# One small VectorE instruction in place of two, in the softmax of an attention stage

## The reference

```python
q_bits = (np.einsum('bhsd,dk->bhsk', q, proj) > 0)      # B, H, S, D = 2, 8, 768, 64; 6 bits
k_bits = (np.einsum('bhsd,dk->bhsk', k, proj) > 0)
mask = q_bucket[:, :, :, None] == k_bucket[:, :, None, :]
scores = np.where(mask, scale * np.matmul(q, k.transpose(0, 1, 3, 2)), -1000000000.0)
scores = scores - np.max(scores, axis=-1, keepdims=True)
attn = np.exp(scores)
attn = attn / (np.sum(attn, axis=-1, keepdims=True) + 1e-09)
return np.matmul(attn, v)
```

## Time and profile before

| | us |
|---|---|
| median of three runs | 738.78 |
| the profiled execution | 738.64 |
| its span, first to last instruction | 736.8 |
| PE busy | 712.6 (97%) |
| DVE busy | 410.8 (56%) |
| ACT busy | 340.2 (46%) |
| POOL busy | 322.7 (44%) |

### The profile page before, as it was taken

How to read it: one execution, slowest core, us unless ns; L and a number is a source line. 1 busy time by engine, 2 the same in 40 slices (tenths; PEclk the granted TensorE clock), 3 DMA queues, 4 the chain that set the end, 5 groups by cost and what they waited for, 6 DMA issues and landing times.

```text
span 736.8 us, 10909 instructions
## 1 busy us (share of the span) xinstructions
PE 712.6 (97%) x3754; PEld 604.0 (82%) x3754; DVE 410.8 (56%) x827; ACT 340.2 (46%) x689; POOL 322.7 (44%) x283
## 2 busy tenths in 40 slices
PE   3999999999999999999999999999999999999998
PEld 2788898889888877888888888888888888888876
DVE  2998899889989587833131122211343556845443
ACT  1899999999999644333101111111233334223101
POOL 3798888878888257955100000020034555121100
PEclk9999999999999999999999999999999999999999
DMA  6464753333332012522000001020011220000002
GB/s 167 115 158 116 179 133 95 104 104 97 95 80 55 1 44 87 152 69 80 1 0 1 1 0 43 2 78 1 1 43 44 86 56 24 1 28 16 15 28 86
DMA packets 39400, 45.77 MB, mean 62 GB/s; under 512 B 15796, under 2 KB 26676, under 8 KB 39348
## 3 DMA queue, kind: packets, MB, share of 16 engines
q1 hardware_dynamic: 36564, 41.65, 20.6%
q0 software_dynamic: 2784, 3.43, 1.8%
HBM read 28.16 MB, written 3.15 MB: 42 GB/s over the span
## 4 chain that ended last, share of the span: by engine, by line
PE 79%; DVE 12%; issue 4%; ACT 2%; DMA 1%; POOL 1%; SPq 1%; ACTq 0%; POOLq 0%; DVEq 0%
PE PS L890 21%; PE PS L892 21%; PE PS L891 21%; DVE negmax L1235 5%; DVE ETL L1244 3%; PE PS L981 3%; PE PS L1021 3%; PE PS L1006 2%; PE PS L1007 2%; PE PS L1022 2%; PE PS L1109 1%; DVE bias L1237 1%; ACT E L775 1%; ACT OS L787 1%; PE PS L992 1%
## 5 line engine op out<-in xcount | busy, mean ns | idle before, releaser
L1387 DVE SCALAR_TENSOR_TENSOR HL<-PS,HH 128x512 fp32r<-128x512 f32 x48 | 33.2, 691 | 154.6 <-ACT HH L876 154.6
L876 ACT ACTIVATE HH<-PS 128x512 fp32r<-128x512 f32 x48 | 28.7, 598 | 181.4 <-PE PS L892 181.4
L1235 DVE TENSOR_REDUCE negmax<-PS 128x1 f32<-128x768 f32 x96 | 91.0, 948 | 28.0 <-PE PS L1007 27.9
L775 ACT ACTIVATE E<-PS,bias,factor 128x768 f32<-128x768 f32 x96 | 95.5, 995 | 21.6 <-DVE factor L1238 15.0
L1244 DVE TENSOR_TENSOR ETL<-PS,ETH 128x384 fp32r<-128x384 f32 x192 | 97.2, 548 | 2.8 <-ACT ETH L768 2.8
L768 ACT ACTIVATE ETH<-PS 128x384 fp32r<-128x384 f32 x192 | 83.1, 485 | 8.2 <-PE PS L981 8.0
L981 PE MATMUL PS<-ident,E 128*128 128x128 f32 x576 | 79.7, 273 | 0.1
L1021 PE MATMUL PS<-ETH,VHL 128*128 128x384 f32 x192 | 72.4, 377 | 4.7 <-ACT OS L787 4.7
L1006 PE MATMUL PS<-TOPH,TOPL 128*128 128x512 f32 x192 | 69.1, 360 | 7.2 <-DMA KM<-MR 6.2
L890 PE MATMUL PS<-UTH,W 128*128 128x512 f32 x192 | 75.8, 395 | 0.2 <-issue 0.2
L892 PE MATMUL PS<-UTH,W 128*128 128x512 f32 x192 | 74.8, 390 | 0.0
(11 more groups left out here) (173 smaller groups left out, 1562.3 us busy)
## 6 DMA issues: line engine op xcount, KB each, us to landing
RAW<-in_moe_w_ch_dram SPq DMA_DIRECT2D x32, 256.0 KB, 2.8
QK<-in_qk_dram SPq DMA_DIRECT2D x16, 384.0 KB, 4.2
QM<-TOPH SPq DMA_DIRECT2D x16, 192.0 KB, 2.9
KM<-TOPL SPq DMA_DIRECT2D x16, 192.0 KB, 3.2
VR<-in_v_dram SPq DMA_DIRECT2D x16, 192.0 KB, 2.7
TOPL<-QM SPq DMA_DIRECT2D x16, 192.0 KB, 2.7
TOPH<-TOPH SPq DMA_DIRECT2D x16, 192.0 KB, 3.0
out_dram<-fin SPq DMA_DIRECT2D x12, 256.0 KB, 2.0
```

The source lines that it names most:

```text
L775: nc.scalar.activation(E[:, tile % NE, :], s_bank(tile)[:, 0:S], ACT.Exp, bias=bias[:, t:t + 1], scale=factor[:, t:t + 1], accum_out=esum[ ...
L1235: nc.vector.tensor_reduce(negmax[:, t:t + 1], s_bank(tile)[:, 0:S], AX_X, ALU.max, negate=True).then_inc(s_max, 1)
```

## The change

`bias` and `factor` become the two columns of one tile, `affine`, and `negmax` gets two columns, of which the first is set to 1.0 once, by a memset on POOL, and the second takes the row maximum. One scalar_tensor_tensor per tile then computes (negmax < PEN/2) * [1.0, negmax], with in0 the maximum repeated and in1 the pair. `s_sb` counts one per tile. DVE waits for the memset once, before the first tile. The tiles take 96 bytes a partition more in all.

```diff
-    negmax = put("negmax", [P, NSTAT])
-    bias = put("bias", [P, NSTAT])
-    factor = put("factor", [P, NSTAT])
+    negmax = put("negmax", [P, NSTAT, 2])
+    affine = put("affine", [P, NSTAT, 2])
...
             pool.wait_ge(s_init, 2)
+            pool.memset(negmax[:], 1.0).then_inc(s_init, 1)
...
-                    act.wait_ge(s_sb, 2 * (tile + 1))
+                    act.wait_ge(s_sb, tile + 1)
...
-                    nc.scalar.activation(E[:, tile % NE, :], s_bank(tile)[:, 0:S], ACT.Exp, bias=bias[:, t:t + 1],
-                                         scale=factor[:, t:t + 1], accum_out=esum[:, t:t + 1]).then_inc(s_exp, 1)
+                    nc.scalar.activation(E[:, tile % NE, :], s_bank(tile)[:, 0:S], ACT.Exp, bias=affine[:, t, 1:2],
+                                         scale=affine[:, t, 0:1], accum_out=esum[:, t:t + 1]).then_inc(s_exp, 1)
...
+                    if tile == 0:
+                        dve.wait_ge(s_init, 3)
                     dve.wait_ge(s_s, tile + 1)
-                    nc.vector.tensor_reduce(negmax[:, t:t + 1], s_bank(tile)[:, 0:S], AX_X, ALU.max, negate=True).then_inc(s_max, 1)
+                    nc.vector.tensor_reduce(negmax[:, t, 1:2], s_bank(tile)[:, 0:S], AX_X, ALU.max, negate=True).then_inc(s_max, 1)
                     dve.wait_ge(s_max, tile + 1)
-                    nc.vector.tensor_scalar(bias[:, t:t + 1], negmax[:, t:t + 1], PEN / 2, negmax[:, t:t + 1], ALU.is_lt, ALU.mult).then_inc(s_sb, 1)
-                    nc.vector.tensor_scalar(factor[:, t:t + 1], negmax[:, t:t + 1], PEN / 2, None, ALU.is_lt).then_inc(s_sb, 1)
+
+                    nc.vector.scalar_tensor_tensor(out=affine[:, t, :], in0=negmax[:, t, 1:2].to_broadcast([P, 2]), scalar=PEN / 2,
+                                                   in1=negmax[:, t, :], op0=ALU.is_lt, op1=ALU.mult).then_inc(s_sb, 1)
```

## The result

The change made the kernel slower: 743.92 us, median of four runs (743.70 to 744.09), against 738.77 for the four of the kernel before run beside them. The ratio is 1.0072, 95% interval 1.0059 to 1.0084; the median is 5.15 us higher. The forecast was slower, 741.0 us in 736.2 to 750. The sign came true, and so did the forecast holds beside POOL's TENSOR_TENSOR; the forecast +2.25 us was less than half of what came, because one kind of hold was left out and the tail was priced too low.

A forecast was written before the change was run, and what follows sets the result against it. PE was taken to bound the kernel, with a 0.47 us hole per head waiting for DVE, then ACT. Middle heads +0.5, first head +0.9, tail +0.45 and +0.4 made +2.25 us: 741.0 us, range 736.2 to 750.

The forecast's parts named there:

- the forecast holds beside POOL's TENSOR_TENSOR: Attention stage: STT, reading two SBUF tensors, waits for a POOL TENSOR_TENSOR under way and ends 0.03 us after it.
- STT, unheld: The small scalar_tensor_tensor on 128x2 elements that replaces bias and factor takes 0.16 us where POOL does not hold it.
- gain at the hole, per head: PE's wait before the matmul that needs OS shrinks from 0.47 to 0.34 us: 0.13 us gained per head.
- later holds (TOPL, VHL): Behind the hole, held STTs delay ETL; PE waits 0.07 and 0.08 us, plus 0.02 from later MR, per head.
- hold by MR at the first place: STT of a head's third tile, beside POOL's MR (TENSOR_SCALAR), was taken as free: no cost.
- first head: DVE sets the pace; STT meets TOPL and VHL, ETL comes 1.1 us late: +0.9 us net.
- tail: Final heads, where POOL does the folds: FE holds STT for +0.45 us, two more such holds give +0.4.
- the fourth place: Place of bias at 128.86, a head's sixth tile: TOPL holds STT 0.9 us in all but first and last heads.
- I take STT as free beside TENSOR_SCALAR: POOL's TENSOR_SCALAR (MR, QK) does not hold STT, since einv inside QK takes 0.17 to 0.21 us.
- The second rival: POOL's TENSOR_SCALAR holds STT too, 2.6 us beside MR; fifteen heads make 37 us, 776 us; chance 0.12.
- The bound of +0.3 per head: Upper bound per middle head if both fifth and sixth places are held, as three later heads have it.
- The third rival: POOL's CAST holds STT at the third place, opening the hole by up to 0.8 us: 750; chance 0.10 with stronger knock-on.

The follow-up runs named there:

- run 1: Changed kernel with in0 of every small STT a column of the scores in PSUM instead of the maximum in SBUF; 736.79 us, ratio 0.9964.
- run 10: Changed kernel with the small STT's first input from PSUM in heads 1 to 13 only, both ends as in the change; 740.13 us, ratio 1.0018.
- run 11: Changed kernel with only the STT of each head's third tile (beside MR) in heads 1 to 13 reading PSUM; 741.96 us, ratio 1.0037.
- run 4: Changed kernel, but POOL starts MR only when the STT of the head's third tile is done; 749.13 us, ratio 1.0135.
- run 9: Changed kernel with the small STT's first input from PSUM in head 0 and heads 14 and 15 only; 739.69 us, ratio 1.0012.
- run 5: Changed kernel plus one 0.15 us one-element tensor_scalar and a wait ahead of the third place's STT, once per head; 754.6 us, ratio 1.0211.
- run 8: Changed kernel with the small STT raising its semaphore by 2 instead of 1, ACT waiting for twice the number; 754.44 us, ratio 1.0213.
- run 2: Kernel before, with bias alone as an STT on 128x1 with two SBUF inputs, factor still a tensor_scalar; 755.54 us, ratio 1.0222.
- run 6: Changed kernel with STT, signalling by 2, only in heads two to fourteen; bias and factor in the first and last two; 750.43 us, ratio 1.0155.
- run 3: Changed kernel with a one-input tensor_scalar on the 128x2 pair in place of STT; 744.16 us, ratio 1.0069.

## Why the prediction came out as it did

Runs 1, 10 and 11 give the middle heads' terms as means over the same thirteen heads (starts of the maxima: 190.18 us before, 192.10 after, 188.28 in run 10, 190.12 in run 11).

| term | forecast | measured | from |
|---|---|---|---|
| STT, unheld | 0.16 us | 0.16 us | run 1 |
| gain at the hole, per head | -0.13 | -0.15 | run 10 less before: -1.90 / 13 |
| later holds (TOPL, VHL) | +0.15 and +0.02 | +0.14 | run 11 less run 10: 1.84 / 13 |
| hold by MR at the first place, with what it brings on | 0 | +0.15, nearly all of it in five heads | after less run 11: 1.98 / 13 |
| first head | +0.9 | +1.10 | the table above |
| tail | +0.85 | +2.53 | the table above |

**Right:** the hold by a TENSOR_TENSOR to 0.03 us after its end; the fourth place, and the fifth and sixth for most heads; the gain; the late ETLs, in run 11 and not in the change, where MR's hold hid them; and the other edits at nothing, since the memset, 0.14 us, changed no start ahead of the stage that can be told from the scatter.

**The step that failed** is "I take STT as free beside TENSOR_SCALAR". It rested on the einv inside QK, 0.17 to 0.21 us long. Two things in the trace of before spoke against it. First, those thirteen einv start 0.64 to 0.68 us after QK, last 0.17 to 0.21, the earlier ones longer, and all end 0.84 to 0.86 after QK's start; the row of 125.48 does. What ends at a fixed distance from another engine's start, however long it takes, is likely released by it: held, but only for what was left of a short stretch. The einv of run 4, held 0.80 and released at 0.85, shows that it was so. Second, one einv of before stands beside a TENSOR_TENSOR. DVE, then POOL:

```profile
227.83 0.63 DVE L1263 TENSOR_SCALAR einv<-esum 128x6 f32<-128x6 f32 x1
```

```profile
227.16 1.27 POOL L590 TENSOR_TENSOR AO<-X 128x512 f32<-128x512 f32 x1
```

It took 0.63 and ended 0.03 after AO: an instruction with one SBUF input is held too, so einv was no witness for a form that can't be held. MR's hold makes STT take 0.50 to 0.84 us in the first fourteen heads of the change, and ends 0.98 to 0.99 after MR's start in each. The second rival, the hold by MR over its full 2.9 us, was wrong in size by far (776 us); truth lay between two cases of which I priced only the ends.

This term fell on the place ahead of the hole. In the six heads with the short hold it changed the path and hardly the time: they lose the gain at the hole instead of losing it behind, and take 14.61 us on average, 0.02 less than before, where the forecast had +0.04. The miss of the middle, +0.5 forecast and +1.92 measured, is the seven heads where the sixth place met `X` or `OS` as well, 0.14 to 0.41 us each. In five of them MR's hold had brought that second hold on (run 11). The bound of +0.3 per head named the pattern, for three heads; the sum went by +0.04 for all thirteen.

**The tail**, +0.85 forecast and +2.53 measured, is the largest miss, and was under-sized for a second reason: I laid STT on POOL's schedule of before (229.56 in FE), while the holds shift the two against each other. With MR at the first place (1.10 us), AO at the second (1.00) and FO at the fourth (1.48), PE waited for ETL four times between 229 and 240 us and once for VHL. Against the unheld form of run 9 the last full head alone (from one third-tile maximum to the next, 227.20 to 244.36 here, 225.23 to 239.53 there) is 17.16 - 14.30 = 2.9 us longer.

The third rival, CAST at the third place, didn't come about, by 0.04 us. Runs 5 and 8 went over that edge and cost 10.7 and 10.5 us against the change; the rival's own 0.8 us in 13 heads make 10.4, not the "up to +9 us" that it gives. Against before, runs 2, 5, 6 and 8 cost 11 to 16 us. Another CAST did hold STT in the change: in five early heads the fifth place stood beside VHL's CAST, took 0.23 to 0.51 us and ended 0.01 after it. The prediction had put those heads' second hold on the sixth place alone.

Of the rule quoted from the Trainium skill, "SBUF — State Buffer", section "SBUF: two separate sides": CAST and TENSOR_TENSOR behave by it, to the end. POOL's TENSOR_SCALAR holds too, as it says, and I set that aside wrongly; but not for the whole instruction as the profile has it: 0.98 of 2.93 us. POOL's spans are rough in the profile; what is shown is when DVE was let go. The section also names a second class, DVE instructions in a two-port performance mode; run 3 and einv fit it, which these runs show by their holds alone. What stays open: why the hold by MR in the tail ends 1.37 after its start (228.17 + 1.10 against 227.90), and not at 0.98; it does so, at 1.36 to 1.38, in every run in which that place is held.

## What to carry to other kernels

Before merging two small VectorE instructions into one with two SBUF inputs, or two elements of one, lay the new instruction over GpSimd's timeline place by place: a 0.1 us gain stands against holds of 0.5 to 1.5 us. Price them together and not one by one: a hold ahead of the critical wait can hide one behind it, and a hold can bring on another one later. Test "not held" by ends, not by lengths, since a short overlap with a hold looks free. Where a start falls within 0.1 us of another engine's, price both sides of the edge, and prefer an edit (immediate for pointer scalar) whose instructions were never held.

## What the runs showed of the hardware

- GpSimd's TENSOR_SCALAR holds VectorE for its first part: beside MR (24x768, 2.93 us) instructions with two inputs or two elements are let go 0.98 us after its start, beside QK (64x768, 2.13 us) the six-element einv at 0.85. Einv that start 0.90 after QK and STTs that start 2.81 after MR are free. Exceptions: the tail's 1.37, and one pair instruction of run 3.
- A VectorE instruction of 128x1 with two SBUF inputs is held (0.75 us beside CAST); one of 128x1 with one tensor never is, with a pointer scalar or without.
- The same two-input instruction with one input in PSUM is never held: 96 times 0.16 us.
- A 128x1 TENSOR_SCALAR with a pointer scalar and two operations takes 0.06 us more than one with an immediate and one operation (214 against 154 ns). The second operation is hardly the cause: STT, with two operations and no pointer, takes 160.
- A semaphore raised by 2 adds an instruction and 0.07 us to the start of the one that carries it.
